# Routed expert tiles of an mLSTM, gMLP and mixture-of-experts kernel: the tile loops written out, with the last tile's finish inside each condition, and fp32 rounding in the routing

## The chip, the cores and the metric

One core of one Trainium2 chip runs the whole program. The metric is the device time of one execution in microseconds. Lower is better.

## The reference, cut to what matters

The first two stages (an mLSTM over 768 steps, then a gated MLP with a spatial product) give x with 2 x 768 tokens of 320 features. The change lies in the third stage, which sends each token to one of 8 experts:

```python
logits = np.einsum('bsd,de->bse', x, w_gate)
local_gate = 1.0 / (1.0 + np.exp(-np.einsum('bsd,de->bse', x, w_local).squeeze(-1)))
for b in range(B):
    prev_e = -1
    for s in range(S):
        fresh_e = int(np.argmax(logits[b, s]))
        if s == 0 or local_gate[b, s] < 0.5:
            e = fresh_e
        else:
            e = prev_e if prev_e >= 0 else fresh_e
        prev_e = e
        ls = logits[b, s] - logits[b, s].max()
        p = np.exp(ls)
        p /= p.sum() + 1e-09
        h = np.maximum(x[b, s] @ w1[e], 0.0)
        out[b, s] = p[e] * (h @ w2[e])
```

w1 is 320 x 1024 and w2 is 1024 x 320 for each expert. A token keeps the expert of the token before it wherever its local gate is open.

## The kernel before

Every engine has a program of its own, written out in order, and they meet only at semaphores (`wait_ge`, `then_inc`). The helper `link` makes the next instruction of the same engine wait for this one.

**Routing.** The 1536 tokens lie in 12 tiles of 128 rows. Small matmuls on TensorE and small operations on VectorE find each token's expert (`oh`, one-hot) and its rank among the expert's tokens (`ranks`). The rank is split into a low digit (rank mod 128, `lo_i`) and a high one (rank div 128, `hi_i`) by int32 shift and mask. `nt` is the number of tiles that each expert needs, from a comparison with the multiples of 128 in `kth`; `tend` is their running sum, so its last entry is the number of tiles in use. `place` marks the tile of each token, `along` multiplies it by token numbers or by the token's weight in three bf16 parts (`weigh`), and the matmuls of `invert` turn this into lists by slot: `gidx` (rows to gather), `sidx` (rows to write), `wtok` (weights). GpSimd sums the exponentials for the softmax meanwhile and writes three registers' worth into `tep`: tiles in use, last tile, tile before it.

**Expert tiles.** Slots are grouped in tiles of 128 with one expert each; NT3 = 19 tiles can occur, NSURE = 12 always do, and the rest depend on the data. GpSimd gathers a tile's rows of x by indirect DMA (`gather`, L691) and scatters its result rows (`scatter`, L699). TensorE does, in `tile_step(j)` (L1940): `up(j, 0)`, `turn_h(j-1, 0)`, `up_last(j)`, `turn_h(j-1, 1)`, `up(j, 1)`, `turn_x(j+1)`, then `down(j-1)`: the first product of tile j (L1899, L1911), the transposes of the hidden values of tile j-1 (L1919), the transpose of the next tile's x (L1880), and the second product of tile j-1 (L1934). fp32 products are made from high and low halves in fp32r (high x high, high x low, low x high). ScalarE writes the high halves (`w1_high` L1000, `w2_high` L1011, `h_high` L1006, `x_high` L990), VectorE most low halves (`w2_low` L1456, `h_low` L1451, `w1_low` L1446, `x_low` L1434), `relu` (L1442) and `result` (L1463), which scales the rows by their weights into `ys`. GpSimd makes three of the four low halves of w1 (L725). The buffers for high and low halves are single or double, so each of these engines waits for TensorE's progress and TensorE for theirs.

**Control.** The expert of a tile is read into a register wherever it is used (`expert`, L363). On ScalarE and VectorE, `over_tiles` (L376) runs tile 1, then a hardware loop with two tiles a round, then another whose halves stand under `If(used > ...)`, and then `finish` for a tile number read from memory:

```python
            with eng.Fori(NSURE // 2, NT3 // 2) as i:
                for odd_ in range(2):
                    with eng.If(used > 2 * i + odd_):
                        step(2 * i + odd_, odd_)
            with eng.If(used > NT3 - 1):
                step(NT3 - 1, 0)
            tail(last_tile(eng))
```

TensorE and GpSimd have their tiles written out, each from 12 on under `If(used > j)`; TensorE then runs `finish(last_tile(pe))` (L1958: both `turn_h`, both `down`), and GpSimd one `If_eq` for each possible count (L749), with the last two scatters and a wait for all of them. While TensorE would be idle in routing, `warm` (L1641) issues matmuls whose result nobody reads.

## Time and profile before

| | |
|---|---|
| three runs | 384.21 us median (382.91 to 388.42) |
| the profiled execution | 381.16 us |
| its span | 379.4 us, so 1.76 us lie around it |
| TensorE matmul busy | 359.3 us, 95% of the span |
| VectorE, ScalarE, GpSimd busy | 75%, 55%, 51% |
| granted TensorE clock, mean | 0.988 |
| tiles in use for these inputs | 15 (15 scatters, L699) |

Times in the views are counted from the start of the span. The chain of waits is followed backwards from the last instruction; "issue" in it is time in which an engine waited for nothing that the profile shows, such as branches and register reads on its sequencer. "PEld" is TensorE's weight load, "PEq", "ACTq", "DVEq", "POOLq" and "SPq" the sequencers.

### The profile page before, as it was taken

To read this page: it belongs to the slowest core of one execution; us is meant where nothing else is said; L and a number is where in the kernel's file an instruction comes from. 1 tells how busy PE (TensorE), PEld (TensorE's weight loads), DVE (VectorE), ACT (ScalarE), POOL (GpSimd) and SP (SyncE) were. 2 spreads that over 40 slices of the span, in tenths; PEclk is the share of its full clock that TensorE was granted. 3 is DMA by queue.
4 is the path that set the end of the run, shared out by engine and by line. 5 is a ranking of instruction groups with operands and counts; after the bars stand their busy time and mean duration, and the time that the engine had idled before them with its cause. 6 is when DMAs were issued, how large, how long until landed. Compare 5 with 4: busy or idle time off the path is not lost.

```text
span 379.4 us, 8028 instructions
## 1 busy us (share of the span) xinstructions
PE 359.3 (95%) x2409; PEld 307.0 (81%) x2409; DVE 283.4 (75%) x535; ACT 208.8 (55%) x456; POOL 195.0 (51%) x220
## 2 busy tenths in 40 slices
PE   8999999999999999999999987899999999999962
PEld 4878999998999899999998644678777878888852
DVE  3899876887786998351566684988889898988940
ACT  3856555556552760243021524777888778878720
POOL 3776455453530403404023567676778777877711
PEclk9999999999999999999999999999999999999968
DMA  8997568756750091002992854984322222211100
GB/s 143 212 215 191 115 145 163 140 124 150 143 166 36 0 331 57 22 0 85 336 397 79 301 167 142 312 338 131 100 69 70 83 65 57 84 36 39 41 6 8
DMA packets 71490, 50.27 MB, mean 132 GB/s; under 512 B 52682, under 2 KB 63211, under 8 KB 71452
## 3 DMA queue, kind: packets, MB, share of 16 engines
q1 hardware_dynamic: 67574, 39.44, 39.6%
q0 software_dynamic: 1808, 5.31, 4.5%
q10 hardware_dynamic: 2070, 5.03, 3.8%
q8 instruction: 21, 0.34, 0.4%
q14 instruction: 17, 0.14, 0.1%
HBM read 45.40 MB, written 4.87 MB: 132 GB/s over the span
## 4 chain that ended last, share of the span: by engine, by line
PE 81%; DVE 7%; DMA 4%; issue 2%; ACT 1%; SPq 1%; POOL 1%; DVEq 1%; ACTq 0%; POOLq 0%
PE psum L1934 14%; PE psum L1734 13%; PE psum L1899 11%; PE psum L1614 6%; PE psum L1814 5%; PE psum L1603 5%; PE psum L1567 5%; PE psum L1911 4%; PE psum L1919 3%; PE psum L1557 3%; DMA heads<-in_q_dram 3%; PE psum L1579 2%; PE psum L1586 2%; PE psum L1880 1%; PE psum L1535 1%
## 5 line engine op out<-in xcount | busy, mean ns | idle before, releaser
L725 POOL TENSOR_TENSOR late<-w1m,late 128x512 fp32r<-128x512 f32 x47 | 64.4, 1386 | 20.1 <-ACT late L1000 19.7
L1456 DVE TENSOR_TENSOR late<-arena,late 128x640 fp32r<-128x640 f32 x60 | 59.3, 1010 | 11.1 <-issue 5.2
L1934 PE MATMUL psum<-late,xt_high_low 128*128 128x320 f32 x300 | 56.4, 321 | 1.5 <-DVE xt_high_low L1451 1.5
L1734 PE MATMUL psum<-halves 128*128 128x384 f32 x288 | 54.5, 340 | 0.0
L1000 ACT ACTIVATE late<-w1m 128x512 fp32r x62 | 39.0, 632 | 26.1 <-PE psum L1899 19.2
L1899 PE MATMUL psum<-late 128*128 128x512 f32 x180 | 50.2, 409 | 2.4 <-ACT late L990 1.2
L1734 PEld LDWEIGHTS psum<-halves 128*128 128x128 f32 x288 | 49.4, 188 | 0.1
L1934 PEld LDWEIGHTS psum<-late,xt_high_low 128*128 128x128 f32 x300 | 47.5, 195 | 2.3 <-DVE xt_high_low L1451 1.9
L1011 ACT ACTIVATE late<-arena 128x640 fp32r x60 | 44.2, 740 | 7.5 <-PE psum L1934 2.7
L1899 PEld LDWEIGHTS psum<-late 128*128 128x128 f32 x180 | 30.8, 188 | 11.5 <-POOL late L725 4.4
L579 POOL TENSOR_SCALAR early<-early 128x320 f32<-128x320 f32 x12 | 12.1, 1012 | 35.4 <-ACT early L815 35.4
L699 POOL DMA_INDIRECT out_dram<-arena x15 | 18.4, 1230 | 20.6 <-DVE arena L1463 20.6
L1344 DVE TENSOR_TENSOR early<-psum,arena 128x384 f32<-128x384 f32 x16 | 8.9, 556 | 25.9 <-PE psum L1734 25.8
L809 ACT ACTIVATE early<-early 128x128 f32<-128x128 f32 x80 | 24.5, 388 | 6.4 <-DMA early<-m_rows 5.6
L1919 PEld LDWEIGHTS psum<-arena 128*128 128x128 f32 x120 | 14.0, 142 | 14.9 <-issue 13.0
L1099 DVE RECIPROCAL early<-early 128x320 f32<-128x320 f32 x12 | 25.7, 2140 | 0.0
L1603 PE MATMUL psum<-halves,xt_high_low 128*128 128x512 f32 x96 | 25.1, 403 | 0.1
L1614 PE MATMUL psum<-xt_high_low,halves 128*128 128x256 f32 x192 | 24.5, 286 | 0.0
L1614 PEld LDWEIGHTS psum<-xt_high_low,halves 128*128 128x128 f32 x192 | 23.3, 191 | 0.6
L549 POOL TENSOR_SCALAR_AFFINE_SELECT early<-early 128x512 f32<-128x512 f32 (+1 forms) x28 | 17.7, 642 | 11.0 <-ACT early L809 10.6
L1567 PE MATMUL psum<-early 128*128 128x41 f32 x192 | 22.8, 279 | 0.0
L1567 PEld LDWEIGHTS psum<-early 128*128 128x128 f32 x192 | 22.4, 192 | 0.4 <-issue 0.4
(276 smaller groups left out, 724.9 us busy)
## 6 DMA issues: line engine op xcount, KB each, us to landing
arena<-in_moe_w_dram SPq DMA_DIRECT2D x8, 1280.0 KB, 7.8
w1m<-in_moe_w_dram SPq DMA_DIRECT2D x8, 1024.0 KB, 10.0
early<-m_rows SPq DMA_DIRECT2D x10, 512.0 KB, 4.7
w_rest<-in_moe_w_dram SPq DMA_DIRECT2D x38, 128.0 KB, 2.8
arena<-in_moe_w_spatial_dram ACTq DMA_DIRECT2D x6, 384.0 KB, 3.8
x_rows<-early SPq DMA_DIRECT2D x12, 192.0 KB, 2.0
heads<-in_q_dram SPq DMA_DIRECT2D x12, 160.0 KB, 4.9
heads<-in_k_dram SPq DMA_DIRECT2D x12, 160.0 KB, 4.4
```

The lines of the kernel that those rows point to most:

```text
L725: g.tensor_tensor(w1l[k % 2], w1m[:, ds(e * 2 * FF + k % 2 * FF + k // 2 * 512, 512)], w1h[k % 2].bitcast(fp32), ALU.subtract).then_inc(m_ ...
L1000: A.activation(w1h[k % 2], w1m[:, ds(e * 2 * FF + k % 2 * FF + k // 2 * 512, 512)], ACT.Copy).then_inc(m_1h, 1)
L1011: A.activation(w2h[:, i * QW:(i + 1) * QW], w2s[:, ds(e * NFT * DM + i * QW, QW)], ACT.Copy).then_inc(m_wh, 1)
L1099: V.reciprocal(sg[b], sg[b]).then_inc(sg_ok[b], 1)
L1456: V.tensor_tensor(w2l[:, i * QW:(i + 1) * QW], w2s[:, ds(e * NFT * DM + i * QW, QW)], w2h[:, i * QW:(i + 1) * QW].bitcast(fp32), ALU.subtr ...
L1567: last = T.matmul(PS[4 * b + 2][:, h * DV:(h + 1) * DV], ep[b][:, h * P:(h + 1) * P], vb[b][:, h, :], start=True, stop=True)
L1603: last = T.matmul(PS[4 * b + 2], x_[:, m, b, :], w_[:, m, FH:F1], start=i == 0, stop=i == len(TERMS) - 1)
L1614: last = T.matmul(to, w_[:, m, dt * P:(dt + 1) * P], x_[:, m, :, :], start=i == 0, stop=i == len(TERMS) - 1)
L1734: last = T.matmul(PS[n % 4][:, 0:HALF], v_[s_][:, dt * P:(dt + 1) * P], w_[half][:, s_ * HALF:(s_ + 1) * HALF], start=s_ == 0 and i == 0, ...
L1899: last = T.matmul(PS[1 + g_], x_[:, m * P:(m + 1) * P], w_[m], start=g_ == 0 and m == 0 and x_ is xsh and w_ is w1h, stop=g_ == 1 and m == ...
L1919: last = T.transpose(PS[3 + g_][:, m * P:(m + 1) * P], hs[:, f:f + P], identf)
L1934: last = T.matmul(PS[5][:, 0:DM], h_[m // 4][:, m % 4 * P:(m % 4 + 1) * P], w_[:, m * DM:(m + 1) * DM], start=m == 0 and h_ is hsh and w_ ...
```

## The change

1. `over_tiles` is written out for all engines: tile 1 to 11 in a row; then, for each possible count j from 12 on, `If_eq(used, j)` holds `finish(j - 1)`, and inside `If(used > j)` stand step j and the same pair for j + 1. `finish` thus knows its tile number when the program is built. Each engine reads the expert of a tile once and keeps the register.
2. TensorE: `down(j-2)` stands at the start of step j instead of `down(j-1)` at the end, the same place in the row; `finish(j)` lays the transposes of the last tile between the halves of `down(j-1)`, and the last tile's own product (`down_last`) goes by operand (four high x high, four high x low, four low x high, for each half) into another bank.
3. VectorE in tile 1: `w1_low(1)` ahead of the third `w2_low(0)`.
4. Routing: high digit and tile counts by adding and subtracting 1.5 x 2^23 (`WHOLE`), which rounds; the low digit of the last three tiles on GpSimd; the sums of the exponentials on VectorE instead of GpSimd, and the weights' split and `along(2, NW)` behind `x_low(0)`.
5. TensorE's fillers: one fewer in routing, two more behind `turn_x(0)`, three behind `turn_x(1)`.

```diff
+        experts = {}
         def expert(eng, j):
+            if not isinstance(j, int):
+                return read_expert(eng, j)
+            if (eng, j) not in experts:
+                experts[eng, j] = read_expert(eng, j)
+            return experts[eng, j]
...
+        def over_tiles(eng, used, step, tail):
+            for j in range(1, NSURE):
+                step(j)
+            def rest(j):
+                with eng.If_eq(eng.to_reg(used), j):
+                    tail(j - 1)
+                if j < NT3:
+                    with eng.If(used > j):
+                        step(j)
+                        rest(j + 1)
+            rest(NSURE)
...
             pool.wait_ge(r_own, TILES_END)
-            for i in range(3):
-                g.tensor_scalar(tep_i[:, NT3 + i:NT3 + i + 1], tend[:, E - 1:E], -float(i), None, ALU.add).then_inc(r_te, 1)
-            pool.wait_ge(r_oh, EXP)
...
+            link(g.tensor_scalar(lo_x, hi_x[:, MOST:NTT], WHOLE, -WHOLE, ALU.add, ALU.add))
+            link(g.tensor_scalar(lo_x, lo_x, -float(P), None, ALU.mult))
+            g.tensor_tensor(lo[:, MOST:NTT], lo_x, rank[:, MOST:NTT], ALU.add).then_inc(r_before, 1)
+            g.tensor_scalar(tep_i[:, NT3:NT3 + 1], tend[:, E - 1:E], 0.0, None, ALU.add).then_inc(r_te, 1)
+            pool.wait_ge(r_one, IN_AT)
...
+            def finish(j):
+                for odd_ in range(2):
+                    pool.wait_ge(d_xs[odd_], 16 * len(range(odd_, min(j + 3, NT3), 2)))
+                scatter(j - 1)
+                scatter(j)
+                pool.wait_ge(d_out, 16 * (j + 1))
...
-            def h_high(j, g_):
-                past(act, m_y, 4 * j)
+            def h_high(j, g_, quarters=None):
+                past(act, m_y, 4 * j if quarters is None else quarters)
...
-                link(V.tensor_scalar(q1.bitcast(i32)[:, n0:n1], rank[:, n0:n1], 0.0, None, ALU.add))
-                link(V.tensor_scalar(hi_i.bitcast(i32)[:, n0:n1], q1.bitcast(i32)[:, n0:n1], 7, None,
-                                     ALU.logical_shift_right))
-                link(V.tensor_scalar(lo_i.bitcast(i32)[:, n0:n1], q1.bitcast(i32)[:, n0:n1], P - 1, None,
-                                     ALU.bitwise_and))
+                link(V.tensor_scalar(hi_x[:, n0:n1], rank[:, n0:n1], 0.5 - P / 2, 1.0 / P, ALU.add, ALU.mult))
...
-            link(V.tensor_tensor(cmpn, kth.unsqueeze(1).to_broadcast([P, E, NTT]),
-                                 count.unsqueeze(2).to_broadcast([P, E, NTT]), ALU.is_lt))
-            link(V.tensor_reduce(nt, cmpn, AXX, ALU.add))
+            ranks(MOST, NTT, COUNT_LAST)
+            link(V.tensor_scalar(nt, COUNTED_ALL, P / 2 - 0.5, 1.0 / P, ALU.add, ALU.mult))
+            link(V.tensor_scalar(nt, nt, WHOLE, -WHOLE, ALU.add, ALU.add))
             V.tensor_tensor_scan(tend, notfirst[:, 1:2].to_broadcast([P, E]), nt, 0.0, ALU.mult, ALU.add).then_inc(r_own, 1)
-            ranks(MOST, NTT, COUNT_LAST)
...
             along(0, 2).then_inc(r_one, 1)
+            dve.wait_ge(r_before, LOW_LAST)
             low_digit(MOST, NTT)
...
-            def tile_step(j, odd_=0):
+            def tile_step(j):
+                if j >= 2:
                     result(j - 2)
-                if later(j):
+                if j == 1:
+                    w1_low(j, expert(dve, j))
+                if j > 0:
                     e = expert(dve, j - 1)
                     w2_low(j - 1, e, 2)
...
             def finish(j):
-                before = tile_before(dve)
-                result(before)
+                result(j - 1)
                 e = expert(dve, j)
-                w2_low(j, e, 2, before)
-                w2_low(j, e, 3, before)
                 h_low(j, 0)
+                w2_low(j, e, 2)
+                w2_low(j, e, 3)
                 h_low(j, 1)
-                result(j)
+                result(j, 1)
...
             def finish(j):
+                down(j - 1, 0)
                 turn_h(j, 0)
+                down(j - 1, 1)
                 turn_h(j, 1)
-                down(j, 0)
-                down(j, 1)
+                down_last(j, 0)
+                down_last(j, 1)
```

How the rows stand, as the built programs list them (line numbers of the changed kernel differ by a few from those before; "[waits ...]" names semaphores).

TensorE, from the end of the last conditional tile step to the start of the last tile's second product, before:

```order
L1969 UNCONDITIONAL_BRANCH
L371 TENSOR_LOAD arena
L371 ISA x2
L346 REGISTER_ALU
L1916 REGISTER_ALU [waits m_htl]
L1919 MATMUL psum<-arena 128x128 [waits m_hs]
L1919 MATMUL psum<-arena 128x128 x3
L1916 REGISTER_ALU [waits m_htl]
L1928 ISA [waits m_hth,m_ys]
L1934 MATMUL psum<-late,xt_high_low 128x320 [waits m_wh]
```

and in the change, from the condition behind a step (L388 is the `If_eq`, L1929 is `down`, L1914 `turn_h`, L1945 `down_last`):

```order
L1875 MATMUL psum<-arena 128x128 [waits m_xs,m_xh,d_xs0]
L388 COMPARE_AND_BRANCH
L1929 MATMUL psum<-late,xt_high_low 128x320 [waits m_wh,m_hth,m_ys]
L1914 MATMUL psum<-arena 128x128 [waits m_hs,m_htl]
L1914 MATMUL psum<-arena 128x128 x3
L1929 MATMUL psum<-late,xt_high_low 128x320 [waits m_wh,m_hth]
L1945 MATMUL psum<-late,xt_high_low 128x320 [waits m_wh,m_hth]
L1945 MATMUL psum<-late,xt_high_low 128x320 [waits m_htl]
L388 UNCONDITIONAL_BRANCH
L391 COMPARE_AND_BRANCH
```

(Rows that continue a group are left out of both.) The register read and the address arithmetic ahead of the transposes are gone, the transposes moved into the product of the tile before, and one condition stands between a step and its finish.

VectorE at the first tiles, from the second low quarter of w2 of tile 0 on, before (L1456 is `w2_low`, L1446 `w1_low`, L1451 `h_low`):

```order
L368 TENSOR_LOAD arena [waits r_te]
L368 ISA x2
L364 TENSOR_LOAD arena
L364 ISA x2
L1456 ISA [waits m_wh]
L1456 TENSOR_TENSOR late<-arena,late 128x640
L1446 ISA [waits m_1h]
L1446 TENSOR_TENSOR late<-w1m,late 128x512
L1451 TENSOR_TENSOR xt_high_low<-psum,xt_high_low 128x512 [waits m_hth]
```

and in the change (L1443 is `w2_low`, L1433 `w1_low`, L1438 `h_low`):

```order
L374 TENSOR_LOAD arena
L374 ISA x2
L1433 ISA [waits m_1h]
L1433 TENSOR_TENSOR late<-w1m,late 128x512
L1443 ISA [waits m_wh]
L1443 TENSOR_TENSOR late<-arena,late 128x640
L1438 TENSOR_TENSOR xt_high_low<-psum,xt_high_low 128x512 [waits m_hth]
```

`w1_low` of tile 1 moved ahead of one `w2_low`, and two of three register reads left this stretch.

## Rows read from the trace of the kernel before

**Rows 1.** The page: TensorE's busy time, and granted clock in 40 slices of the span.
```profile
PE 359.3 (95%) x2409; PEld 307.0 (81%) x2409; DVE 283.4 (75%) x535; ACT 208.8 (55%) x456; POOL 195.0 (51%) x220
...
PEclk9999999999999999999999999999999999999968
```

**Rows 2.** Chain that ended last, from 348.87 us: start, duration (us), what.
```profile
348.87 3.52 PE psum L1934 x24
...
355.27 0.59 PE psum L1919 x4
...
357.65 3.51 PE psum L1934 x24
361.16 2.15 issue
363.31 0.68 PE psum L1919 x4
...
366.47 0.69 DVE xt_high_low L1451
...
367.21 5.05 PE psum L1934 x22
...
372.50 0.56 DVE arena L1463
373.33 0.97 POOL out_dram L699
```

**Rows 3.** Busy time by stretch: length, each engine (count), granted clock, DMA share, GB/s.
```profile
320.00:340.00 20.00, 20.00 (x118) 16.06 (x117) 18.24 (x26) 16.06 (x28) 15.09 (x11) 1.00 0.21 61
...
363.30:367.20 3.90, 2.41 (x10) 1.62 (x10) 2.80 (x5) 1.82 (x3) 1.39 (x1) 0.57 0.00 0
367.20:370.60 3.40, 3.39 (x13) 3.39 (x14) 0.56 (x1) 0.00 (x0) 0.00 (x0) 0.50 0.03 10
```

**Rows 4.** The page's costliest groups: ScalarE's and VectorE's halves of w2.
```profile
L1456 DVE TENSOR_TENSOR late<-arena,late 128x640 fp32r<-128x640 f32 x60 | 59.3, 1010 | 11.1 <-issue 5.2
...
L1011 ACT ACTIVATE late<-arena 128x640 fp32r x60 | 44.2, 740 | 7.5 <-PE psum L1934 2.7
```

**Rows 5.** The scatters: time from issue to landing.
```profile
DMA to landing us min/median/max: 2.2/2.7/6.1
```

**Rows 6.** Instructions in order of time, tiles 0 to 2: start, duration, engine, what, idle before.
```profile
232.08 0.69 DVE L1446 TENSOR_TENSOR late<-w1m,late 128x512 fp32r<-128x512 f32 x1 [1.50 <-ACT late L1000]
...
239.38 1.54 POOL L725 TENSOR_TENSOR late<-w1m,late 128x512 fp32r<-128x512 f32 x1 [0.23 <-ACT late L1000]
239.70 1.77 DVE L1446 TENSOR_TENSOR late<-w1m,late 128x512 fp32r<-128x512 f32 x1
241.52 0.50 PE L1899 MATMUL psum<-late 128*128 128x512 f32 x1 [0.80 <-DVE late L1446]
...
248.58 1.30 POOL L699 DMA_INDIRECT out_dram<-arena  x1 [1.22 <-DVE arena L1463]
...
251.26 0.30 PEld L1899 LDWEIGHTS psum<-late 128*128 128x128 f32 x2 [0.51 <-POOL late L725]
```

**Rows 7.** VectorE in routing, after the last counts, and one GpSimd operation beside it.
```profile
218.54 0.26 DVE L1379 TENSOR_TENSOR early<-arena,psum 128x96 f32<-128x96 f32 x1 [0.54 <-PE psum L1785]
...
219.12 0.17 DVE L1382 TENSOR_TENSOR_SCAN early<-early 128x8 f32<-128x8 f32 x1
...
219.62 0.19 DVE L1328 TENSOR_SCALAR early<-early 128x3 int32<-128x3 f32 x1
...
220.26 0.17 DVE L1385 SCALAR_TENSOR_TENSOR early<-early 128x8 f32<-128x8 f32 x1
...
222.27 0.63 DVE L1335 TENSOR_TENSOR early<-early 128x384 bf16<-128x384 bf16 x1
...
226.34 0.87 DVE L1393 TENSOR_TENSOR arena<-early,arena 128x684 bf16<-128x684 bf16 x1
...
220.89 0.27 POOL L712 TENSOR_SCALAR early<-early 128x12 f32<-128x12 f32 x1
```

171 lines of the change are left out of this document (75 added, 96 removed).

## The prediction

> **What bounds the kernel now.** I read the page first. TensorE's matmuls cover 95% of the span and its granted clock is full (2.4 GHz) in every slice but the last two [rows 1]. So a saving counts only where TensorE stands idle, and there are few such places. The busy time by stretch says the same of the tiles in full swing: 20.00 us busy in 20.00 us, with VectorE at 18.24, ScalarE at 16.06 and GpSimd at 15.09 [rows 3]. The chain of waits shows a tile there as matmuls end to end, and the reader can take the pitch from it: the second product of one tile starts at 348.87, that of the next at 357.65, 8.78 us later [rows 2]. Nothing that the change does to ScalarE, VectorE or GpSimd can shorten these tiles; it can only lengthen them.
>
> The chain then shows where TensorE does stand idle. At 361.16 the next to last product ends and 2.15 us of "issue" follow: four conditions for tiles that aren't in use, and the read of the last tile's number. Then come the transposes, a chain through ScalarE and VectorE to h_low (L1451, ends about 367.16), and 22 matmuls in 5.05 us that need 0.147 us each (3.52 / 24) at full clock [rows 2]. The stretch view says why they are slow: the granted clock was 0.57 and then 0.50, the lower level of 1.2 GHz, after the idle time [rows 3]. The instructions in order of time show two smaller stalls at tiles 1 and 2 [rows 6]. In routing TensorE has only fillers, and VectorE's chain sets the pace [rows 7].
>
> **The end (edit 1 with `finish` on all engines).** The changed end starts at 357.65, behind turn_x: first half of down(13), transposes, second half, transposes, last product. At the pitches of the chain that is 3.51 + 2 x 0.59 + 24 x 0.147 = 8.22 us, so it ends at 365.9, against 367.21 + 5.05 = 372.3 before [rows 2]. Gain 6.4 us. The others must keep up, so I follow them. ScalarE: the third w2 quarter can go when the third quarter of down(13) is done, at 357.65 + 1.76 + 0.59 + 0.88 = 360.9; then 0.74 us for it [rows 4], h_high, the fourth quarter and h_high again. Even if each takes 0.74, the two high halves are there at 362.4 and 363.9. TensorE wants them at 362.4 and 364.1. VectorE: result(13) from 361.9 (0.56), h_low (0.69) to 363.2, then two low quarters to 364.8 if they take the 0.8 that they take without GpSimd beside them, or 365.2 at their mean of 1.01 [rows 4], h_low again to 365.4 or 365.9. TensorE wants the first h_low at 363.5 and the last at 365.3. So 0.1 to 0.6 us may be waited. I take -6.3. Ends: -6.4, and -3.0 if the last result waits for a transfer (below).
>
> **The tail behind the last scatter.** It is issued at 373.33 [rows 2] and the span ends at 379.4, 6.1 us later; it lands some 2.7 us after issue [rows 5]. In the 3.4 us left, GpSimd passes four `If_eq` that don't hold; in the change it jumps once to the end. If four conditions and a read took TensorE 2.15 us [rows 2], one costs about 0.4, and the row understates it, as TensorE's queue ran on in the meantime. Three fewer: I take -1.0. Ends: -1.6, and +2.1, if the one long jump costs by itself what the whole issue row shows.
>
> **Three skipped finishes.** At 12, 13 and 14 every engine now jumps over a `finish` that isn't its own. Before, TensorE's conditions there held and nothing shows of them: pitch unchanged. A jump of 0.4 us or more meets engines that have work queued: TensorE waits for GpSimd's low half in the middle of up(j, 1) and then has about 0.8 us of matmuls issued. I take +0.3 in all. Ends: 0, and +6.4 (three times the issue row of 2.15). The Trainium skill ("Advanced Engine Details and Errata", Control Flow Timing) gives about 108 ns for a compare-and-branch; the 2.15 us row for four and a read does not agree, and by that price, as an estimate, this term would be nothing and the tail -0.3.
>
> **Tiles 1 and 2 (edit 3, and the register reads).** At 239.38 GpSimd starts its low half of w1, and VectorE's w1_low, queued from 239.70, ends only at 241.47: 1.77 us, with both operands in SBUF, where h_low takes 0.69 [rows 2, 6]. It seems to wait until GpSimd is done (240.92). TensorE stalls 0.80 us for it [rows 6]. In the change it comes one low quarter (0.8 us) and two register reads earlier, so before GpSimd's start, and the stall goes. What is late next is the w2_low put behind it: blocked until 240.9, it ends near 241.6, h_low near 242.3, and down(0) now wants h_low at about 242.4. It just fits. In tile 2 TensorE's loads stall 0.51 us for GpSimd (251.26), which waited for VectorE's result(0) before the scatter at 248.58 [rows 6]; with TensorE 0.8 us earlier, this wait could grow instead of going, as GpSimd's gather and scatter stand in front. Both gone is -1.3, only the first moved into the second is 0. I take -1.0.
>
> **Routing (edit 4).** On VectorE after the last counts, the comparison and reduction (218.54 to 219.12, 0.58 us) become two small operations at about 0.21: -0.16. The three integer steps (219.62 to 220.26, 0.64) become one: -0.43 [rows 7]. The scan now stands right ahead of its reader instead of five operations before it: +0.1. The low digit of the last tiles goes to GpSimd: three linked operations of 0.27 or less [rows 7], 1.1 us from the scan with the waits between them, and is wanted 2.0 us after it (as from L1385 at 220.26 to L1335 at 222.27 before). Covered. The softmax sums come to VectorE behind `sidx`, when it waits for the gather anyway. The weights' split, four steps of about 0.2 and an `along` of 0.87 [rows 7], so 1.7 us, now stands between x_low(0) and w1_low(0), where VectorE is idle for 1.5 us [rows 6]; TensorE asks for it after up_last(0), about when it is ready. GpSimd's four satisfied waits behind IN_AT: +0.05. Sum -0.45. Ends: -0.6, and +0.5 if the weights come late. Fillers stand in idle TensorE time (one fewer, five more, 0.22 us each): 0.
>
> **Sum.** -6.3 - 1.0 + 0.3 - 1.0 - 0.45 = -8.45 us, against the profiled execution of 381.16 (span 379.4): 372.7, a factor of 0.978. On the median of the runs, 384.21, the same factor gives 375.7.
>
> **The rivals.**
> *A transfer takes the wait's place.* result(14) writes `ys` only when scatter(13) has landed. Now the scatter goes out at about 362.8 and result(14) is ready at 366.1. At the median of 2.7 us it has landed, at the maximum of 6.1 [rows 5] it lands at 368.9, and 2.8 us of the gain go. For it: less than a microsecond of room over the median. Against: little other traffic then, 10 GB/s and less in the last stretches [rows 3]. Total -5.6: 378.5 on the median.
> *The start gives nothing.* The early w1_low only brings TensorE sooner to the wait for GpSimd. For it: that order of GpSimd is unchanged and the 0.51 us stall shows that it is on the edge [rows 6]. Total -7.4: 376.7.
> *Branches cost more than the end gives.* The place is behind steps 11, 12 and 13, on the engines whose code moved, and at the very end on GpSimd. If each of three skips costs TensorE the whole 2.15 us of the issue row, that is +6.4, and with +2.1 in the tail instead of -1.0 the sum is -6.3 + 6.4 + 2.1 - 1.0 - 0.45 = +0.8 us: 385.0, slower than before. It decides from about 1.9 us a jump. For it: the issue row is long for what it holds [rows 2], and ScalarE and VectorE leave short loops for long written-out code. Against: a finish is short beside the four whole steps that the 2.15 us skipped, and written-out TensorE code ran without gaps in full swing [rows 3]. The Trainium skill ("Runtime: NRT & Kernel Launch", Instruction fetch mechanics) says that a taken branch to a target outside the fetched window stalls for a DMA; no row here shows a single jump alone.
>
> **How the numbers follow.** Forecast 0.52, start gives nothing 0.20, transfer 0.14, branches 0.14. A measurement of this kernel can tell about 2% from no change, 7.7 us of 384.21. The forecast, -8.5, lies only 0.8 us beyond it, so I count 0.42 of its 0.52 as faster, and 0.08 of the second case; with 0.02 from a better tail that makes 0.52 faster. Slower by over 2% needs jumps of over 4 us each: 0.04. Within: 0.44. The range: low is all good ends, -6.4 - 1.6 - 1.3 - 0.6 = -9.9, and 0.6% for a median of few runs: 372.0. High is between the transfer case (378.5) and the branch case (385.0): 381.0, which leaves part of the latter out.
>
> **What would show it.** Right: no issue row over 1 us in the chain near the end; L1929 and L1945 without a gap from turn_x on; granted clock at full until the last matmul; last product done some 8.2 us after the last turn_x; w1_low of tile 1 at 0.7 us and no 0.80 stall; the time from the last counts to the first gather 0.4 us shorter. Wrong: gaps in TensorE before down(10), down(11) or down(12) (branches); VectorE's last result waiting for a DMA (transfer); TensorE waiting for GpSimd's L720 in tile 2 by a microsecond (start). The forecast fails as a whole if the tile pitch is no longer 8.78 us.

## The result, and the profile after

The changed kernel takes 372.89 us (median of 6 runs, 371.38 to 376.4) beside 383.74 us for the kernel before on the same chip (6 runs): a ratio of 0.9728, 95% interval 0.9675 to 0.9781. Run once more among the last experiments it gave 372.24 us and 0.9696 (0.9666 to 0.9727). That is 10.9 and 12.1 us less than the kernel before beside it, where 8.5 were predicted; both medians are in the predicted range (372.0 to 381.0), but just above its lower end and some 3 us below the predicted time.

The page of the changed kernel, TensorE's busy time and granted clock, and VectorE's low halves of w2. It answers to [rows 1] and [rows 4]:

```profile
PE 356.7 (96%) x2413; PEld 307.7 (83%) x2413; DVE 282.3 (76%) x536; ACT 207.3 (56%) x455; POOL 190.1 (51%) x212
...
PEclk9999999999999999999999999999999999999998
...
L1443 DVE TENSOR_TENSOR late<-arena,late 128x640 fp32r<-128x640 f32 x60 | 59.0, 1002 | 8.6 <-ACT late L1001 6.8
```

The clock is full up to the last slice; the slice at 6 is gone. Now the chain that ended last (start, duration in us, what), to be laid beside [rows 2]:

```profile
348.13 3.52 PE psum L1929 x24
...
356.85 1.76 PE psum L1929 x12
358.61 0.44 PE psum L1914 x4
359.04 0.89 PE psum L1929 x6
...
360.15 0.54 issue
360.69 0.59 ACT xt_high_low L996
...
361.32 3.80 PE psum L1945 x24
...
365.97 0.97 POOL out_dram L702
```

The 2.15 us of issue are gone. The last transposes lie between the two halves of the next to last product, and the last product does 24 matmuls in 3.80 us where before 22 took 5.05. From the end of the last turn_x (356.85, before 357.65) to the end of the last matmul it is 8.27 us; before 14.61 (357.65 to 372.26). The chain passes once through ScalarE (360.69), with TensorE still at its transposes beside it. The busy time by stretch says why the matmuls keep their pace, with the columns of [rows 3] (the granted clock is the third number from the end):

```profile
320.00:340.00 20.00, 20.00 (x118) 16.45 (x117) 18.18 (x26) 15.77 (x29) 14.50 (x12) 1.00 0.21 61
...
356.85:361.00 4.15, 4.15 (x32) 4.13 (x31) 3.60 (x6) 3.31 (x7) 2.54 (x2) 1.00 0.01 4
361.00:365.10 4.10, 4.01 (x27) 3.52 (x24) 3.06 (x5) 1.38 (x3) 1.38 (x1) 1.00 0.05 15
```

TensorE has no idle time before 361, and its clock stays at the upper level (1.00) to the last matmul. Before, in the stretch with the idle time, it was 0.57 and then 0.50 [rows 3].

The instructions in order of time, tiles 0 to 2, beside [rows 6]:

```profile
239.49 0.68 DVE L1433 TENSOR_TENSOR late<-w1m,late 128x512 fp32r<-128x512 f32 x1
...
239.87 1.45 POOL L720 TENSOR_TENSOR late<-w1m,late 128x512 fp32r<-128x512 f32 x1 [0.19 <-ACT late L990]
...
240.09 1.90 DVE L1443 TENSOR_TENSOR late<-arena,late 128x640 fp32r<-128x640 f32 x1
...
251.24 0.73 PE L1894 MATMUL psum<-late 128*128 128x512 f32 x2 [0.52 <-POOL late L720]
251.24 0.30 PEld L1894 LDWEIGHTS psum<-late 128*128 128x128 f32 x2 [0.96 <-POOL late L720]
```

w1_low of tile 1 takes 0.68 us instead of 1.77, and it is the w2_low behind it that is now long (1.90). The 0.80 us stall is gone, but the one in tile 2 has grown. The 0.51 us of [rows 6] is the idle time of the weight load, and the like number is now 0.96. The matmuls of that product had no gap before, and stand in one row:

```profile
250.02 1.97 PE L1899 MATMUL psum<-late 128*128 128x512 f32 x6
```

By the chains down(0) starts 13.03 us after the first turn_x, before 14.39, which is 1.36 us gained; from down(0) to down(1) it is then 9.56 us (242.74 to 252.30), before 9.05 (243.27 to 252.32), so 0.51 of it is lost again. An ordinary tile takes about 8.7.

VectorE in routing, from the last counts to `gidx`, and the first gather on GpSimd, beside [rows 7]:

```profile
220.68 0.18 DVE L1316 TENSOR_TENSOR early<-psum,early 128x24 f32<-128x24 f32 x1 [0.54 <-PE psum L1780]
...
225.23 0.17 DVE L1392 TENSOR_SCALAR arena<-early 128x19 int32<-128x19 f32 x1
...
225.71 1.25 POOL L694 DMA_INDIRECT arena<-x_rows,arena  x1 [2.66 <-DVE arena L1392]
```

The last counts are there at 220.68, before at 218.54 [rows 7]: 2.14 us later, in a part of the program that the change doesn't touch. So the profiled executions (373.6 beside 381.16) show only 7.6 us of the gain. Counted from the last counts to the end of the span, it is 160.86 us before and 150.92 after. This is how that divides (us, each between two instructions of the same meaning in the two traces):

| stretch | before | after | difference | forecast |
|---|---|---|---|---|
| last counts to the end of `gidx` | 5.39 | 4.72 | -0.67 | -0.5 |
| end of `gidx` to the first turn_x | 4.95 | 4.31 | -0.64 | +0.05 |
| first turn_x to the start of down(1) | 23.44 | 22.59 | -0.85 | -1.0 |
| down(1) to the end of the last turn_x | 105.33 | 104.55 | -0.78 | +0.3 |
| that to the end of the last matmul | 14.61 | 8.27 | -6.34 | -6.3 |
| that to the last scatter | 1.07 | 0.85 | -0.22 | in the row above |
| last scatter to the end of the span | 6.07 | 5.63 | -0.44 | -1.0 |
| sum | 160.86 | 150.92 | -9.94 | -8.45 |

The start of the first turn_x is taken from the chain, which begins a matmul that waits for nothing at the end of the one in front of it (229.71 in the changed kernel, where its own row begins at 229.55). By its own row the second and third differences would be -0.80 and -0.69, with the same sum. All times after the first turn_x below are counted by the chain.

Two rows had to be explained by runs, because the forecast had nothing there: the 0.64 us in front of the first turn_x, and the 0.78 us in tiles that I had said nothing could shorten.

### The profile page after: what moved, and what is told of

Same layout as the page of the kernel before. It is cut to its first block, busy times and chain, and to the rows that moved or that the text cites. A ratio compares the mean times of both kernels' runs of the same rounds, so it can differ in the third digit from the quotient of the medians.

```text
span 371.6 us, 7371 instructions
## 1 busy us (share of the span) xinstructions
PE 356.7 (96%) x2413; PEld 307.7 (83%) x2413; DVE 282.3 (76%) x536; ACT 207.3 (56%) x455; POOL 190.1 (51%) x212
## 4 chain that ended last, share of the span: by engine, by line
PE 81%; DVE 7%; ACT 3%; DMA 3%; issue 2%; SPq 1%; POOL 1%; DVEq 0%; POOLq 0%; ACTq 0%
PE psum L1729 13%; PE psum L1929 13%; PE psum L1894 10%; PE psum L1609 5%; PE psum L1809 5%; PE psum L1598 5%; PE psum L1906 4%; PE psum L1562 4%; PE psum L1914 4%; PE psum L1552 3%; PE psum L1574 2%; PE psum L1581 2%; PE psum L1639 2%; DMA early<-m_rows 1%; PE psum L1875 1%
## 5 line engine op out<-in xcount | busy, mean ns | idle before, releaser
L720 POOL TENSOR_TENSOR late<-w1m,late 128x512 fp32r<-128x512 f32 x47 | 61.3, 1319 | 20.8 <-ACT late L990 20.7
L1443 DVE TENSOR_TENSOR late<-arena,late 128x640 fp32r<-128x640 f32 x60 | 59.0, 1002 | 8.6 <-ACT late L1001 6.8
L1929 PE MATMUL psum<-late,xt_high_low 128*128 128x320 f32 x280 | 50.9, 313 | 0.0
L1894 PE MATMUL psum<-late 128*128 128x512 f32 x180 | 49.1, 405 | 1.0 <-POOL late L720 0.8
L1929 PEld LDWEIGHTS psum<-late,xt_high_low 128*128 128x128 f32 x280 | 42.8, 188 | 0.0
L1894 PEld LDWEIGHTS psum<-late 128*128 128x128 f32 x180 | 31.7, 188 | 8.6 <-POOL late L720 2.5
L583 POOL TENSOR_SCALAR early<-early 128x320 f32<-128x320 f32 x12 | 12.1, 1011 | 34.9 <-ACT early L807 34.9
L702 POOL DMA_INDIRECT out_dram<-arena x15 | 19.9, 1324 | 13.9 <-DVE arena L1450 13.9
L1914 PEld LDWEIGHTS psum<-arena 128*128 128x128 f32 x120 | 13.8, 140 | 12.5 <-issue 10.6
```

The lines of the kernel that those rows point to most:

```text
L720: g.tensor_tensor(w1l[k % 2], w1m[:, ds(e * 2 * FF + k % 2 * FF + k // 2 * 512, 512)], w1h[k % 2].bitcast(fp32), ALU.subtract).then_inc(m_ ...
L1443: V.tensor_tensor(w2l[:, i * QW:(i + 1) * QW], w2s[:, ds(e * NFT * DM + i * QW, QW)], w2h[:, i * QW:(i + 1) * QW].bitcast(fp32), ALU.subtr ...
L1894: last = T.matmul(PS[1 + g_], x_[:, m * P:(m + 1) * P], w_[m], start=g_ == 0 and m == 0 and x_ is xsh and w_ is w1h, stop=g_ == 1 and m == ...
L1914: last = T.transpose(PS[3 + g_][:, m * P:(m + 1) * P], hs[:, f:f + P], identf)
L1929: last = T.matmul(PS[5][:, 0:DM], h_[m // 4][:, m % 4 * P:(m % 4 + 1) * P], w_[:, m * DM:(m + 1) * DM], start=m == 0 and h_ is hsh and w_ ...
```

## The experiments

Unless said otherwise each is the changed kernel with one edit. "To the end" is the time from the last counts to the end of the span, 150.92 in the changed kernel and 150.98 when it was run again; it leaves the differing start out.

**1. The finish in its old order, in its new place.** How much of the end is the overlap, and how much that the finish is written out in each condition?

```diff
             def finish(j):
                 down(j - 1, 0)
-                turn_h(j, 0)
                 down(j - 1, 1)
+                turn_h(j, 0)
                 turn_h(j, 1)
-                down_last(j, 0)
-                down_last(j, 1)
+                down(j, 0)
+                down(j, 1)
```

The same on ScalarE (the first h_high waits for the whole product) and VectorE (h_low behind the third quarter of w2, the last result from the usual bank).

> The changed kernel with the last tile's finish in the order of before (whole down(j-1), both transposes, down(j) in bank 5; ScalarE and VectorE in the old order), but still written out behind its condition. If the overlap of the finish is what gave most of the end, TensorE waits again behind the last transposes (transpose 0.6, h_high 0.6, h_low 0.7 and the quarter of w2: about 3 us), and the clock may fall after it: the stretch from the last turn_x to the last product's end goes from 8.3 us to 11.3 or more. If the conditions and the read of the last tile number were the main cost, it stays below 10.3 (8.3 plus at most 2): before it was 14.6. Ratio to before 0.979 to 0.984 in the first case, 0.975 in the second.

376.52 us, ratio 0.9826 (0.9759 to 0.9893); 154.56 us to the end. From the last turn_x to the last matmul it is 11.91 us, between 8.27 and 14.61. The chain of this run, and its busy time by stretch:

```profile
359.13 0.89 PE psum L1914 x8
...
361.09 0.82 DVE late L1443
361.92 0.61 DVE xt_high_low L1438
...
362.57 4.95 PE psum L1929 x22
```

```profile
360.00:364.00 4.00, 1.96 (x8) 1.72 (x8) 2.79 (x5) 1.37 (x3) 1.01 (x1) 0.80 0.04 11
364.00:367.60 3.60, 3.51 (x19) 3.24 (x17) 0.06 (x1) 0.00 (x0) 0.00 (x0) 0.75 0.02 5
```

There is no issue row of 2 us here, and still TensorE waits from 360.0 to 362.57 for the chain through ScalarE and VectorE, and the 22 matmuls behind it take 4.95 us at a clock between the levels (0.80 and 0.75 on average). So the end has two parts: 2.70 us come from the finish standing in its condition, with no skips and no read ahead of it, and 3.64 us from the new order of the finish, which covers the wait and with that keeps the clock up. (The edit takes back the overlap and the order by operand in the last product together; they were not separated. And the 2.70 is counted from the old end of one profile, 14.61, which is the shortest of three; see experiments 10 and 11. The interval of the ratio is wide; the 3.64 us are read from the two traces.)

**2. More skips.** A `finish` under a condition that never holds behind each of tiles 1 to 11, on every engine.

```diff
             for j in range(1, NSURE):
                 step(j)
+                with eng.If_eq(eng.to_reg(used), NT3):
+                    tail(j)
```

> The changed kernel with one more finish behind each of tiles 1 to 11, under a condition that doesn't hold (count = 19), on every engine: 11 more skipped finishes. If a skipped block costs TensorE nothing while it has work queued, the pitch of a tile stays at 8.7 us and the ratio at 0.973. If a jump costs 0.4 us in the open, 11 of them add 4.4 us (pitch 9.1, ratio 0.984). If each fetches code by a transfer (2 us), they add 20 us or more, and the kernel is slower than before.

372.45 us, ratio 0.9724 (0.9656 to 0.9792). Eleven more skips, and a tile still takes some 8.7 us and the chain has matmuls end to end. It is 104.74 us from down(1) to the last turn_x instead of 104.55, so 0.19 us for eleven, not far from the 104.44 to 104.62 of the other versions that have no stall there. 151.52 us to the end, of which 6.05 lie behind the last scatter instead of 5.63. So while TensorE has work queued a skip costs its chain some 0.02 us at most, and not the 0.4 us that I had set for one. The Trainium skill ("Advanced Engine Details and Errata", Control Flow Timing) gives about 108 ns for a compare-and-branch; by that price eleven would be 1.2 us, as an estimate, so most of it is hidden here and this run can't test the figure. Nor does it say what a skip costs with nothing queued, as in the issue row of 2.15 us: what in that row are the conditions and what the read was not separated.

**3. Each expert read where it is used.** The memory of `expert` is taken out, so that the number is read into a register at each use, as before; in a second run on GpSimd alone.

```diff
         def expert(eng, j):
-            if not isinstance(j, int):
-                return read_expert(eng, j)
-            if (eng, j) not in experts:
-                experts[eng, j] = read_expert(eng, j)
-            return experts[eng, j]
+            return read_expert(eng, j)
```

> The changed kernel with the expert's register read at every use on all engines, as before, instead of once for each tile and engine. The tile pitch went from 8.78 to 8.71 us with the change. If the extra reads on GpSimd made its low half of w1 late, the pitch is 8.78 again (up to 0.1 more), 0.7 to 1 us in all. Rival: the hardware loop and its dynamic addresses on VectorE and ScalarE cost it; then the pitch stays at 8.71.

> The changed kernel with the expert's register read at every use on GpSimd alone. If GpSimd's reads are the cause of the 0.07 us a tile, the pitch is 8.78 here as well. If it is 8.71, and higher in the run with all engines' reads, it is VectorE or ScalarE.

All reads back: 374.11 us, ratio 0.9779 (0.9698 to 0.986), 151.82 us to the end. On GpSimd alone: 371.77 us in one run, 150.83 to the end. The pitch is 8.71 and 8.70, so the reads are not what made it 8.78. But the first of them shows the transfer rival of the prediction at work, in the chain at its end:

```profile
361.85 3.45 DMA out_dram<-arena
...
365.40 0.56 DVE arena L1446
...
366.23 0.97 POOL out_dram L698
```

The last result starts when the scatter before it has landed, 3.45 us after it went out; the last scatter comes 9.75 us after the last turn_x instead of 9.12. In the changed kernel the same scatter goes out at 362.23, and the result (365.14) waits for the matmul. There, it landed in under 2.9 us. The room is a few tenths of a microsecond. Why it landed later here was not found; in the other profiled runs with one `ys` and the new finish the last result waited for the matmul.

**4. The order of GpSimd's waits ahead of the first gather.** The changed kernel waits for the index list (`IN_AT`) first and then passes four waits for x's rows, which hold by then. Here the four stand first again and the wait for the list last, right ahead of the gather, as before.

```diff
-            pool.wait_ge(r_one, IN_AT)
             for t in range(NX2):
                 pool.wait_ge(d_x2[t], 16 * (NTT // NX2))
+            pool.wait_ge(r_one, IN_AT)
```

> The changed kernel with GpSimd's four waits for the stored x rows ahead of the wait for the gather indices again, as before. From the end of VectorE's index operation to the start of the first gather it took 0.93 us before and 0.31 us with the change. If the order of the waits makes this, it is 0.9 again here. Rival: GpSimd's shorter work ahead of it makes it; then 0.3.

One run, 372.19 us; 151.28 to the end. The gather starts 0.93 us after `gidx` again, as before, and in the changed kernel 0.31 us after it. (All profiles show one or the other: 0.29 to 0.31 us with the changed order, 0.92 to 0.94 with the old.) So the order alone is worth 0.62 us, and not in the way one would guess: the gather is late where the wait for the list is the last thing ahead of it, and the four satisfied waits cost nothing that shows where they stand between the two. The chains of this run and of the kernel before have an issue row of 0.85 us between the end of that wait and the gather; what GpSimd does in it was not found. But turn_x(0) starts only 0.17 us later, 4.48 us after `gidx` beside 4.31. TensorE in order of time says why: the fillers and the first turn_x in the kernel before, in this run, and in the changed kernel.

```profile
223.05 5.12 PE L1644 MATMUL psum<-arena 128*128 128x512 bf16 x23
228.88 0.55 PE L1880 MATMUL psum<-arena 128*128 128x128 f32 x3 [0.71 <-DMA arena<-x_rows,arena]
```

```profile
222.73 5.12 PE L1639 MATMUL psum<-arena 128*128 128x512 bf16 x23
228.02 0.55 PE L1875 MATMUL psum<-arena 128*128 128x128 f32 x3 [0.16 <-DMA arena<-x_rows,arena]
```

```profile
224.59 5.12 PE L1639 MATMUL psum<-arena 128*128 128x512 bf16 x23
229.55 0.49 PE L1875 MATMUL psum<-arena 128*128 128x128 f32 x3
```

Before, TensorE is done with its 23 fillers and waits 0.71 us for the gathered rows; here 0.16; in the changed kernel nothing is awaited, and turn_x(0) follows the last filler. The fillers in front of turn_x(0) now set the start, and some of them could go. (Those were not among the five that experiment 6 takes out, and it was not tried.) Where turn_x(0) doesn't wait, up(0) also follows it in 0.80 us instead of 1.02, so at up(0) the order of the waits is worth 0.17 + 0.22, some 0.4 us (it starts 5.11 us after `gidx` instead of 5.50). The other part of the shorter way is that turn_x(0) came 3.55 us after the gather here, against 4.02 before (3.94 and 4.20 in experiments 10 and 11). Why the rows landed sooner was not found.

**5. w1_low of tile 1 late again.**

```diff
                 if j >= 2:
                     result(j - 2)
-                if j == 1:
-                    w1_low(j, expert(dve, j))
                 if j > 0:
                     e = expert(dve, j - 1)
                     w2_low(j - 1, e, 2)
-                if j != 1:
-                    w1_low(j, expert(dve, j))
+                w1_low(j, expert(dve, j))
```

> The changed kernel with VectorE's w1_low of tile 1 behind the third low quarter of w2 of tile 0 again. If the early place gave the gain of tile 1, TensorE stalls about 0.8 us in up(1, 1) again, and the first down(0) comes 0.8 us later after the first turn_x (13.8 instead of 13.0 us), while GpSimd's wait in tile 2 takes up part of it, so that down(1) comes only 0.3 later. Rival: fewer register reads gave it; then 13.0 to 13.3.

One run, 374.41 us; 151.58 to the end. VectorE and GpSimd in order of time:

```profile
240.01 1.57 POOL L720 TENSOR_TENSOR late<-w1m,late 128x512 fp32r<-128x512 f32 x1 [0.20 <-ACT late L990]
...
240.37 1.76 DVE L1433 TENSOR_TENSOR late<-w1m,late 128x512 fp32r<-128x512 f32 x1
```

The long w1_low of [rows 6] is back, 1.76 us, ending 0.5 us behind GpSimd's operation. down(0) starts 14.10 us after the first turn_x (13.03 in the changed kernel) and down(1) at 23.27 (22.59). The early place is worth 1.07 us at first, where 0.8 had been expected, and 0.68 us one tile on, where 0.3 had been. The difference goes into the stall in tile 2, which is smaller here than in the changed kernel (0.64 us at the weight load instead of 0.96).

**6. The fillers of the third stage taken out** (three in tile 0, two behind the first turn_x).

```diff
-                if j == 0:
-                    warm(3, unit, 3)
...
-            warm(2, unit, 3)
```

> The changed kernel without the five filler matmuls behind turn_x(0) and turn_x(1). They stand where TensorE waits anyway. If they cost nothing and give nothing, up(0, 0) starts 0.8 us and down(0) 13.0 us after turn_x(0) as with them. If they are late (they end just as ScalarE's copy does), up(1, 0) starts up to 0.1 us sooner without them. If they hold the clock up, the granted clock falls below 1 in 229 to 245 us and the matmuls there slow down.

One run, 371.94 us; 150.97 to the end, and every stretch as in the changed kernel. These five do nothing. The 23 in front of the first turn_x stay.

**7. The stall in tile 2.** GpSimd's w1_low(2, 3) ahead of the first scatter, since in [rows 6] GpSimd waits 1.22 us for result(0) with that low half behind it.

```diff
                 if j + 2 < NT3:
                     gather(j + 2)
+                if j == 2:
+                    w1_low(j, 3)
                 if j >= 2:
                     scatter(j - 2)
-                w1_low(j, 3)
+                if j != 2:
+                    w1_low(j, 3)
```

> The changed kernel with GpSimd's fourth low half of w1 of tile 2 ahead of the first scatter instead of behind it. If the scatter's wait for result(0) is what makes TensorE wait 0.52 us in tile 2, that wait goes and the first down(1) comes 0.5 us sooner after the first turn_x (22.1 instead of 22.6 us). Rival: the half is late because its high half is, and nothing moves. In the time 0.5 us at most, below what three rounds tell.

371.72 us, ratio 0.9687 (0.9623 to 0.9751); 150.96 to the end, as without it. down(1) starts 21.78 us after the first turn_x instead of 22.59, so the stall in tile 2 is gone, and it was worth 0.81 us, not the 0.5 expected from the matmuls' idle time; but the next tile takes 9.59 us. VectorE in order of time, and TensorE's stall:

```profile
254.63 0.55 DVE L1453 TENSOR_SCALAR arena<-psum,arena 128x320 f32<-128x320 f32 x1 [0.77 <-DMA out_dram<-arena]
...
258.19 0.74 PE L1897 MATMUL psum<-late 128*128 128x512 f32 x2 [0.62 <-POOL late L720]
```

result(1) has to wait until scatter(0) has landed, as both use the one buffer `ys`; behind it come scatter(1) and the low half that TensorE wants. The stall has moved one tile on.

**8. Two result buffers.** Experiment 7 with a second `ys` and a second semaphore, so that result(j) waits for scatter(j - 2).

```diff
-                    bounds_check=bound, oob_is_err=False).then_inc(d_out, 16)
+                    bounds_check=bound, oob_is_err=False).then_inc(d_out[j % 2], 16)
...
-                past(dve, d_out, 16 * j)
-                V.tensor_scalar(ys, PS[bank][:, 0:DM], wtok[:, ds(j, 1)], None, ALU.mult).then_inc(m_ys, 1)
+                past(dve, d_out[j % 2], 16 * (j // 2))
+                V.tensor_scalar(ys[j % 2], PS[bank][:, 0:DM], wtok[:, ds(j, 1)], None, ALU.mult).then_inc(m_ys, 1)
```

> The changed kernel with tile 2's GpSimd order as in the run e6_scatter_behind (the low half of w1 ahead of the first scatter) and two result buffers, so that result(j) waits for scatter(j-2) and not for scatter(j-1); 216 words more SBUF and a second semaphore. Theory: the stall of tile 3 in e6 was VectorE's result(1) waiting for the landing of scatter(0). With two buffers it is gone: the second tile's first matmul 21.8 us after the first turn of x as in e6 (22.6 in the changed kernel), the tile after it at the ordinary 8.71 to 8.8 instead of 9.59, pitch 8.71, the end 8.3 us as in the changed kernel, so 0.8 us less than the changed kernel, ratio to before about 0.970 beside 0.9728. Rival: the stall is GpSimd's share of the port or its queue (the scatter's own 1.4 us of issue lies somewhere in any case), and moves to a later operation again: then tile 3 or 4 is again 0.5 to 0.9 us longer and the total is that of the changed kernel.

The theory held for the tiles: down(1) at 21.77 us, the next tile 8.72 us, and result(1) without a wait:

```profile
255.25 0.54 DVE L1455 TENSOR_SCALAR arena<-psum,arena 128x320 f32<-128x320 f32 x1
```

It is 150.48 us to the end, 0.44 less than the changed kernel, where 0.8 had been expected. The tiles give the 0.8; 0.28 go behind the last scatter (5.91 us instead of 5.63), for which no run shows a cause. In the time of whole runs it doesn't show: 372.33 us, ratio 0.971 (0.9678 to 0.9742), beside 372.24 and 0.9696 for the changed kernel in the same batch. So this version is not shown to be faster. By its code the last result no longer waits for the scatter just before it, so the transfer rival should be gone with it.

**9. The changed kernel again.**

> The changed kernel itself, once more, beside e8, e9 and e12 on one chip: ratio to before 0.972 to 0.974 expected, pitch 8.71, 8.3 us from the last turn of x to the last matmul. It also shows how far the start of the program (routing's last counts at 220.68 us in the changed kernel's profile, 218.54 in that of before) differs from execution to execution: if that is chance it comes nearer 218.5 to 219.5; if the change causes it, it stays at 220.7.

372.24 us, ratio 0.9696 (0.9666 to 0.9727). The stretches come again within 0.06 us: 22.58 us to down(1), 104.55 from there to the last turn_x, 8.27 to the last matmul, 5.69 behind the last scatter. The last counts come at 222.32 us, even later than 220.68. The change doesn't cause it, as the next run shows, which has the old code up to there.

**10. and 11. The kernel before, with loops written out.** What made a tile 8.78 us? In the first, the loops of ScalarE and VectorE are written out, in the second ScalarE's alone. The finish keeps its place and its order.

```diff
-            step(1, 1)
-            with eng.Fori(1, NSURE // 2) as i:
-                step(2 * i, 0)
-                step(2 * i + 1, 1)
-            with eng.Fori(NSURE // 2, NT3 // 2) as i:
-                for odd_ in range(2):
-                    with eng.If(used > 2 * i + odd_):
-                        step(2 * i + odd_, odd_)
-            with eng.If(used > NT3 - 1):
-                step(NT3 - 1, 0)
+            for j in range(1, NSURE):
+                step(j, j % 2)
+            for j in range(NSURE, NT3):
+                with eng.If(used > j):
+                    step(j, j % 2)
```

> The kernel before, with only ScalarE's and VectorE's tile loops written out (a step for each tile with constants in place of the loop's register, conditions from tile 8 on kept, the finish still reading its tile's number). Theory: the loop and the addresses that it computes are what put the 0.2 to 0.4 us of issue time before VectorE's w2_low in each tile, and so the tile pitch 8.78 us. Then the pitch falls to 8.71 (8.70 to 8.73), from the second tile's first matmul to the last turn of x 104.6 us instead of 105.3, and the end stays: 14.6 us from the last turn of x to the last matmul (14.0 to 14.8). Total against before: ratio about 0.996 to 0.998. Rival: the pitch comes from the register reads per tile or from something in the finish's code; then it stays at 8.78 (8.76 to 8.79). Second rival: the written-out finish alone made the end short through the waits of the loop's conditions; then the 14.6 would fall by over 1 us here.

> The kernel before, with only ScalarE's tile loop written out and VectorE's left. If VectorE's loop alone makes the pitch (its issue gap before w2_low pushes its w1_low into GpSimd's operation), the pitch stays at 8.77 to 8.78. If ScalarE's loop makes it (its late high halves hold VectorE), the pitch falls to 8.71. If both share it, something between, 8.73 to 8.76. The end stays at 14.6 us from the last turn of x to the last matmul in every case.

Both written out: from tile 3 on the steps of TensorE's chain are 8.68 to 8.72 us, and it is 104.46 us from down(1) to the last turn_x, as in the changed kernel (104.55) and not as before (105.33). ScalarE's alone: 105.14 us, steps from 8.69 to 8.82. So the pitch comes from the loops, and most of the gain is there only with VectorE's gone too (VectorE's alone was not run). The groups of VectorE and GpSimd from 260 to 350 us (count, busy us, mean ns, idle before and what ended it), first of the kernel before, then of the changed kernel, then with both loops written out, then with ScalarE's alone:

```profile
L1456 DVE TENSOR_TENSOR late<-arena,late 128x640 fp32r<-128x640 f32 x41 | 41.3, 1026 | 7.7 <-ACT late L1011 3.5 <-issue 3.5
...
L725 POOL TENSOR_TENSOR late<-w1m,late 128x512 fp32r<-128x512 f32 x31 | 43.0, 1400 | 13.1 <-ACT late L1000 12.7
```

```profile
L1443 DVE TENSOR_TENSOR late<-arena,late 128x640 fp32r<-128x640 f32 x41 | 39.6, 984 | 6.6 <-ACT late L1001 5.0 <-issue 0.5
...
L720 POOL TENSOR_TENSOR late<-w1m,late 128x512 fp32r<-128x512 f32 x32 | 41.3, 1304 | 15.0 <-ACT late L990 14.9
```

```profile
L1451 DVE TENSOR_TENSOR late<-arena,late 128x640 fp32r<-128x640 f32 x43 | 41.1, 975 | 7.1 <-ACT late L1006 6.9 <-issue 0.2
...
L720 POOL TENSOR_TENSOR late<-w1m,late 128x512 fp32r<-128x512 f32 x30 | 38.7, 1305 | 12.8 <-ACT late L995 12.8
```

```profile
L1465 DVE TENSOR_TENSOR late<-arena,late 128x640 fp32r<-128x640 f32 x41 | 40.8, 1012 | 8.4 <-issue 3.9 <-PE psum L1943 2.1 <-ACT late L1020 2.0
...
L734 POOL TENSOR_TENSOR late<-w1m,late 128x512 fp32r<-128x512 f32 x31 | 43.7, 1424 | 12.8 <-ACT late L1009 12.0 <-issue 0.3
```

With its loop, VectorE loses 3.5 to 3.9 us of "issue" over some ten tiles ahead of w2_low, in time in which nothing is awaited; without it, 0.2 to 0.5. And GpSimd's low half of w1, whose code no one changed, takes 1.40 to 1.42 us on average with VectorE's loop, and 1.30 without. TensorE waits for that low half in up(j, 1), whose six matmuls take longer where it comes late. From the chains of the kernel before and of the changed kernel:

```profile
303.14 1.46 PE psum L1899 x6
```

```profile
346.42 1.38 PE psum L1894 x6
```

The view of waits for the same 90 us bears this out (time in all, how often, longest). TensorE's weight loads of that product wait for GpSimd's low half ten times in the kernel before, once in the changed kernel, and seven times (1.7 us) with ScalarE's loop alone written out; with both written out the view has no such row. The kernel before and the changed kernel:

```profile
PEld psum L1899 <- POOL late L725: 2.4, 10, 0.3
```

```profile
PEld psum L1894 <- POOL late L720: 0.3, 1, 0.3
```

So it is shown that the loops make this low half late, and the matmuls with it. That VectorE's delay pushes its own operations into GpSimd's is read from the four pairs of groups above; that step was not tried by itself, and the loop's branches and the addresses worked out from its register were not separated.

In whole runs neither gains: 384.26 us, ratio 1.0007 (0.9978 to 1.0036), and 384.12 us, 0.9994 (0.9971 to 1.0017). The 0.9 us of the first lie within the interval (0.3% is 1.1 us), and part is given back at the end, where the last 22 matmuls took 5.80 us, and 6.25 us with ScalarE's loop alone written out, instead of 5.05 [rows 2]. The chain's end with both loops written out:

```profile
361.92 3.51 PE psum L1929 x24
365.44 1.69 issue
...
371.02 5.80 PE psum L1929 x22
```

From the last turn_x to the last matmul that makes 14.89 and 16.01 us, where I had expected 14.6. Writing out the loops alone doesn't shorten the end, and the old end has no fixed length: it depends on how long the clock stays down behind the gap. With ScalarE's loop alone written out the granted clock is 0.50 from 368 to 374 us and 0.62 on average from 374 to 378; in the kernel before it is 0.50 up to 370.6 and the product ends at 372.26. Whether that is chance or belongs to these kernels, one profile of each can't say.

These two runs also show the start. The kernel before and the one with both loops written out have the same code up to the last counts. Yet in the latter they come 5.0 us later than in [rows 7] (VectorE in order of time), with a granted clock of 0.83 instead of 1.00 in the first 20 us:

```profile
223.54 0.25 DVE L1374 TENSOR_TENSOR early<-arena,psum 128x96 f32<-128x96 f32 x1 [0.54 <-PE psum L1780]
```

```profile
0.00:20.00 20.00, 16.72 (x102) 13.35 (x103) 9.26 (x26) 9.46 (x27) 7.90 (x24) 0.83 0.95 169
```

Over all profiled executions it ranges from 218.4 to 223.5 us, for either kernel. The clock is not all of it: in experiment 8 the clock was 1.00 there, and the counts came at 220.32. What else it is stays open. A difference of a few microseconds between two single profiles says nothing, unless the start is taken out.

## Why the prediction was right, and where it was wrong

**The end, right.** -6.3 forecast, -6.34 measured, and by the mechanism that was named: 8.27 us against the 8.22 worked out, no wait for a transfer, the clock at its upper level to the end. That the last product took 3.80 instead of 3.52 is the 0.1 to 0.6 us allowed for; that the sum still came out to 0.05 us is partly luck, as the transposes took 0.44 us each and not 0.59. Experiment 1 divides the gain: 3.64 for the new order of the finish and 2.70 for its place. The 0.22 us from the last matmul to the last scatter come beside it; I had not counted them.

**The tail, sign right, size wrong.** I took -1.0 from "one costs about 0.4", a quarter of the issue row. It was -0.44. Where the term failed is that price, which no run showed on GpSimd. The versions of the changed kernel have 5.60 to 6.05 us there, the kernel before and the two of experiments 10 and 11 have 6.07 to 6.16, so the two groups nearly touch, and no run shows the cause of the 0.44.

**Three skipped finishes, too dear.** +0.3 forecast; by experiment 2, with 0.19 us for eleven, three are 0.05. The rival "branches cost more than the end gives" falls with it, and with it the chance of slower. The Trainium skill's stall for a taken branch outside the fetched window ("Runtime: NRT & Kernel Launch", Instruction fetch mechanics) did not show: with every engine skipping a finish after each tile 0.19 us in all reached TensorE's chain. A finish is short, and whether any of these jumps left the window is not known, so no run here tests that rule.

**Tiles 1 and 2, right, between the two ends.** -0.85 against -1.0. The 0.80 us stall went as worked out, and w2_low took over the blocked time (1.90 us). I had written that the wait in tile 2 "could grow instead of going", and it grew: 1.36 us were gained up to down(0) and 0.51 lost from there to down(1). So the rival "the start gives nothing" came true by more than a third, and -1.0 is near the measured value because the first gain was larger than the 0.80 us stall. And 0.22 us of the gain are up(0) coming sooner after the first turn_x, which is a matter of the start and not of this term. So the term's own size is nearer 0.65, much as in experiment 5 (0.68).

**Routing, half of it missed.** VectorE's part was right: -0.67 to the end of `gidx` against -0.5, and GpSimd's digit and the weights' split were covered as forecast. But I had set "GpSimd's four satisfied waits behind IN_AT: +0.05". The place was right and the sign was not: with the wait for the list ahead of the four instead of behind them the gather starts 0.62 us sooner (experiment 4). I had priced only the waits that come to stand behind it, and not what lay between the wait for the list and the gather before. Of the 0.6 us, 0.4 arrive at up(0), since the fillers take over as what turn_x(0) comes behind; another 0.5 us are rows that landed sooner, unexplained.

**The tiles in full swing, wrong step.** "Nothing that the change does to ScalarE, VectorE or GpSimd can shorten these tiles; it can only lengthen them." They became 0.07 us shorter each, 0.78 in all. I took TensorE's 20.00 of 20.00 us busy for a bound by TensorE alone. Matmuls whose operand is a little late show as longer ones, not as a gap: six of them in 1.46 us where 1.38 is possible. The loops were behind it, and most of it is there only with VectorE's gone (0.19 us of the 0.87 with ScalarE's alone written out; experiments 10 and 11). By my own words the forecast "fails as a whole" if the pitch is no longer 8.78; this was too strong, as the pitch moved by less than one per cent and the other terms stood.

**The transfer rival, real but not here.** It did not occur in the changed kernel, and occurred in the first run of experiment 3 at 0.6 us instead of 2.8, alone of the profiled runs with that end and one `ys`. The chance of 0.14 was fair for a margin this thin.

In all: -8.45 forecast, -9.94 measured from the last counts on. The miss of 1.5 us is 0.7 from in front of the first turn_x, 1.1 from the pitch and the skips, and 0.6 the other way from the tail, with the rest in small terms. The medians give 10.9 and 12.1 us; the old end with its varying length may be the rest, as its one profile (14.61) is the shortest of three (14.89 and 16.01).

## What to carry to other kernels

At the end of a kernel an idle TensorE costs twice: the gap, and the matmuls behind it at the lower clock. Put independent work of the tile before into the gap, and let each engine find its last tile in the condition it is already in. Before you call a stretch bound by TensorE because it is busy all the time, compare the duration of the same group of matmuls from tile to tile: an operand that comes a little late hides there, and its cause may be another engine's loop. Removing a stall at one tile is only worth it if you follow the buffer behind it: here it moved one tile on, until the result had a second buffer.

## What the runs showed of the hardware that I had not expected

- GpSimd's indirect DMA started 0.93 us after its index list where the wait for the list stood right ahead of it, and 0.31 us where four waits that already held stood between the two.
- A hardware loop over tiles, with addresses from its register, left VectorE 0.35 to 0.4 us a tile without work and without anything awaited; eleven skipped conditional blocks in written-out code cost TensorE 0.19 us in all.
- The same 22 matmuls behind the same kind of gap took 5.05, 5.80 and 6.25 us: how long the clock stays at its lower level differed between three profiled executions, each of another kernel with the same TensorE code there.
- VectorE's subtraction of two operands in SBUF, 0.68 us alone for 512 elements a row, took 1.76 us where GpSimd's own such subtraction ran beside it, and that for 640 elements 1.90 us instead of 0.81; they ended 0.5 to 0.7 us behind GpSimd's.
- The same scatter landed in under 2.9 us and in 3.45 us, at the same place of two kernels that differ only in when they read the expert.
- A wait can hide in a busy TensorE: weight loads that waited ten times, 2.4 us in all, lengthened its matmuls and left no gap between them (20.00 us busy of 20.00).
